# Three edits to the expert routing of a fused attention, gated FFN and expert kernel: second tile gathered early, second expert fixed early, router matrix turned once

## The reference

```
x = attention(q, k, v)            # 4 batches x 8 heads, 576 tokens, block-causal mask (blocks of 64)
x = (sigmoid(x @ w_gate) * (x @ w_val)) @ w_out        # 512 -> 1536 -> 512
logits = x @ router                                     # 2304 x 8
expert_idx = argmax(logits)
gate_w = softmax(logits)[expert_idx]
for e in range(8):
    mask = expert_idx == e
    h = maximum(x[mask] @ w1[e], 0)                     # 512 -> 1024
    out[mask] = gate_w[mask] * (h @ w2[e])              # 1024 -> 512
```

## Time and profile before

| what | us |
|---|---|
| median of 3 runs | 953.57 |
| the profiled execution | 957.25 |
| its span, first to last instruction | 955.5 |
| PE busy | 899.2 (94%) |
| DVE / ACT / POOL busy | 515.7 / 298.2 / 273.7 |
| mean granted PE clock | 0.976 of 2.4 GHz |

### The profile page before, as it was taken

The page is one execution under the profiler, slowest core; times in us unless marked ns, Lnnn a source line. Parts: engine busy times, 40 slices in busy tenths (PEclk is TensorE's granted clock), DMA queues, the critical chain, the costliest instruction groups (busy, mean ns, idle before and its releaser), DMA issues.

```text
span 955.5 us, 15628 instructions
## 1 busy us (share of the span) xinstructions
PE 899.2 (94%) x5198; PEld 742.0 (78%) x5199; DVE 515.7 (54%) x1027; ACT 298.2 (31%) x672; POOL 273.7 (29%) x254
## 2 busy tenths in 40 slices
PE   7989898999999999999999999799878999989995
PEld 3545454589999999999999999698667888878884
DVE  5777676741248549638747746933543435362241
ACT  4555455532231121121122112123132424351140
POOL 4133335321112213212212212123043435452242
PEclk9999999999999999999999999899798999989998
DMA  4544455422230020010002000022144336382130
GB/s 133 160 158 159 157 171 165 146 95 78 77 122 1 1 67 1 1 34 34 1 1 67 1 1 34 28 94 85 51 168 149 130 132 210 113 276 70 44 132 28
DMA packets 48089, 85.29 MB, mean 89 GB/s; under 512 B 9247, under 2 KB 21535, under 8 KB 47904
## 3 DMA queue, kind: packets, MB, share of 16 engines
q1 hardware_dynamic: 42272, 69.32, 22.1%
q0 software_dynamic: 3360, 10.50, 3.4%
q10 hardware_dynamic: 2400, 4.72, 1.4%
HBM read 70.28 MB, written 14.76 MB: 89 GB/s over the span
## 4 chain that ended last, share of the span: by engine, by line
PE 73%; DMA 8%; DVE 7%; issue 5%; POOL 2%; ACT 2%; SPq 1%; POOLq 0%; DVEq 0%; ACTq 0%
PE bank L1383 21%; PE bank L1385 20%; PE bank L1384 20%; DMA rinv_scratch<-rinv 3%; PE bank L1355 3%; PE bank L1316 3%; PE bank L1328 3%; DMA rwide<-rinv_scratch 2%; PE bank L1518 2%; POOL w1l L436 2%; DVE yT L1021 2%; DMA stage<-in_we 2%; DVE bank L1021 1%; DVE nmax L971 1%; PE bank L1486 1%
## 5 line engine op out<-in xcount | busy, mean ns | idle before, releaser
L689 POOL TENSOR_TENSOR hl<-hraw,hh 128x384 fp32r<-128x384 f32 x72 | 93.7, 1302 | 366.4 <-ACT hh L826 366.4
L1383 PE MATMUL bank<-xh,w1h 128*128 128x384 f32 x576 | 195.6, 340 | 2.0 <-DVE hraw L1143 2.0
L1385 PE MATMUL bank<-xh,w1l 128*128 128x384 f32 x576 | 194.5, 338 | 0.0
L1384 PE MATMUL bank<-xl,w1h 128*128 128x384 f32 x576 | 194.3, 337 | 0.0
L1143 DVE TENSOR_TENSOR hraw<-hraw,bank 128x384 f32<-128x384 f32 x72 | 39.8, 553 | 178.8 <-ACT hraw L871 178.3
L1383 PEld LDWEIGHTS bank<-xh,w1h 128*128 128x128 f32 x576 | 109.4, 190 | 4.8 <-DVE hraw L1143 2.5
L1384 PEld LDWEIGHTS bank<-xl,w1h 128*128 128x128 f32 x576 | 109.4, 190 | 2.2
L1385 PEld LDWEIGHTS bank<-xh,w1l 128*128 128x128 f32 x576 | 109.2, 190 | 0.0
L797 ACT ACTIVATE prob<-bank,nmax 128x576 f32<-128x576 f32 (+2 forms) x144 | 75.9, 528 | 89.4 <-DVE nmax L971 86.4
L871 ACT ACTIVATE hraw<-bank 128x384 f32<-128x384 f32 x72 | 35.4, 491 | 216.3 <-PE bank L1385 216.3
L1021 DVE CUSTOM_DVE_ANT_0 yT<-yrow,wrb 128x512 f32<-128x512 f32 x60 | 89.3, 1488 | 0.0
(11 more groups left out here) (184 smaller groups left out, 1420.5 us busy)
## 6 DMA issues: line engine op xcount, KB each, us to landing
stage<-in_we SPq DMA_DIRECT2D x56, 512.0 KB, 4.4
w1raw<-in_w SPq DMA_DIRECT2D x8, 768.0 KB, 4.6
kt<-in_kT SPq DMA_DIRECT2D x16, 288.0 KB, 3.4
qt<-in_qT SPq DMA_DIRECT2D x16, 288.0 KB, 3.8
rwide<-rinv_scratch SPq DMA_DIRECT2D x32, 144.0 KB, 3.0
xt_scratch<-xo SPq DMA_DIRECT2D x16, 288.0 KB, 2.2
xraw<-xt_scratch SPq DMA_DIRECT2D x6, 768.0 KB, 4.6
y_scratch<-yrow ACTq DMA_DIRECT2D x6, 768.0 KB, 5.0
```

What stands on the lines that cost most here:

```text
L689: pool.tensor_tensor(hl[:, f % 2, :], hraw[:, f % 2, :], hh[:, f % 2, :].bitcast(F32), ALU.subtract).then_inc(h_low, 1)
L1383: pe.matmul(out_, wh, ah, start=first, stop=False, skip_group_check=True)
L1384: pe.matmul(out_, wh, al, start=False, stop=False, skip_group_check=True)
L1385: return pe.matmul(out_, wl, ah, start=False, stop=last, skip_group_check=True)
```

## The change

1. **Router matrix turned once.** wrb becomes [8, 512]. In group 0 SP loads four pieces of 128x1024 (one after each of the w_out blocks 7 to 10) into the still unused yrow, and POOL copies each into wrb with the two axes exchanged, in steps 8 to 11 (`wrb_turn`). Each piece waits for the copy of the one before, as they share one place.
2. **One dense order of routing** for all groups: logits 3, 3, 6, 6, 6 in steps 0 to 4, `routes` in 5, `ranks` in 6, `slots` in 7, `table` in 8, `add_table` in 9. So `first_expert` (17 small operations instead of 13) moves from step 10 of group 4 to step 7.
3. **Second tile early.** After group 4's tokens are in the table, the first expert's second column is looked up too (`first_rows(1)`), and POOL gathers tile 1 in step 10 of group 5. Its rows get their own split buffers ygh1 and ygl1. Should the expert have fewer than 256 rows by then, the column stays as it is and later rows go to the next one (`filled`).
4. **Second expert fixed early** as the first of the ascending order; its weights are requested right behind those of the first one. It gets at least one tile.
5. **The start of the expert part is written out** for tiles 0 and 1, in halves (`up_half`), with matmuls of tile 1 in the places where PE waited for tile 0's hidden rows; ACT does both relus there.
6. **In `over_loads`** the eighth block of the next load moves behind the load's second tile (`second_step`), or into an Else branch where there is none (`rest`).

```diff
-    NT = TT + E - 1
+    NT = TT + E
-        wrb = sb(s2, "wrb", [P, D, E])
+        wrb = sb(s2, "wrb", [P, E, D])
-        def route_steps(G):
-            if G == G_LAST:
-                return [0, 4, 8, 16, 24], 4, 5, 6, 7
-            return [3 * f for f in range(9)], 8, 9, 10, 11
+        LOGIT_STEP = [0, 3, 6, 12, 18, 24]
+        HOT_STEP, RANK_STEP, SLOT_STEP, TAB_STEP = 5, 6, 7, 8
+        ROWS0_STEP, GATHER1_STEP = 9, 10
...
+                if WRB_STEP <= k < WRB_STEP + 4:
+                    j = k - WRB_STEP
+                    if j:
+                        sp.wait_ge(wrb_made, j)
+                    sp.dma_start(yrow[:].rearrange("p m d -> p (m d)")[:, 0:WD * E],
...
+            def wrb_turn(j):
+                pool.wait_ge(wrb_loaded, 16 * (j + 1))
+                pool.tensor_copy(wrb[:, :, j * WD:(j + 1) * WD],
+                                 yrow[:].rearrange("p m d -> p (m d)")[:, 0:WD * E].rearrange("p (d e) -> p e d", e=E)
+                                 ).then_inc(wrb_made, 1)
...
                     hlow(G, f)
+                    if G == 0 and WRB_STEP < f <= WRB_STEP + 4:
+                        wrb_turn(f - WRB_STEP - 1)
                     if G == G_LAST:
                         if f == 1:
+                            early_gather(0)
                         weights_low(pool, 0, 0, LOW_POOL_STEP.get(f, []), ew_low_p)
+                        if f == GATHER1_STEP:
+                            early_gather(1)
             pool.wait_ge(second_known, 1)
-            pool.wait_ge(ygT_done, 1)
+            pool.wait_ge(ygT_done, 2)
...
-            gather(1)
+            gather(2)
+            weights_low(pool, 1, 1, LOW_POOL[:2], ew_low_p)
             pool.wait_ge(tables, 1)
             columns(0)
-            pool.wait_ge(tables, 2)
-            gather_ahead(0)
+            gather_ahead(1)
+            scatter(1)
+            pool.wait_ge(out_stored, 16)
+            columns(1)
...
-                    dve.tensor_tensor_reduce(junk, yrow[:, m, :], wrb[:, :, e], 1.0, 0.0, ALU.mult, ALU.add,
+                    dve.tensor_tensor_reduce(junk, yrow[:, m, :], wrb[:, e, :], 1.0, 0.0, ALU.mult, ALU.add,
...
+            up_half(0, 0, [0, 1])
             for m in range(GM):
                 turn_y(GM * G_LAST + m, m)
+            turn_rows(1)
             for m in range(GM):
                 router(m)
-            expert_up(0, 0, 0)
+            up_half(0, 0, [2, 3]).then_inc(el1_half, 1)
+            up_half(0, 1, [0, 1])
+            ranks(G_LAST)
+            up_half(0, 1, [2, 3]).then_inc(el1_done, 1)
+            pe.wait_ge(yg_high, 2)
+            pe.wait_ge(yg_low, 2)
+            pe.wait_ge(hrow_a, 1)
+            up_half(1, 0, [0, 1])
             turn_hidden(0)
+            up_half(1, 0, [2, 3])
             table(G_LAST)
+            up_half(1, 1, range(C)).then_inc(el1_done, 1)
             expert_down(0, 0, 1)
-            turn_rows(1)
+            turn_rows(2)
+            turn_hidden(1)
             pe.wait_ge(loads_known, 1)
-            over_loads(pe, first_step, step)
+            over_loads(pe, first_step, step, step)
```

More of the change, by code:

```diff
@@ L436, in weights_low, with over_loads, from_second @@
                 eng.tensor_tensor(lo, stage_at(k), h.bitcast(F32), ALU.subtract).then_inc(made, 1)
[L438 removed]
+        def over_loads(eng, first_step, second_step, step, rest=None):
+            def from_second(l, par, t, t1):
+                with eng.If(t1 > t):
+                    second_step(l, par, t)
+                    with eng.If(t1 > t + 1):
+                        with eng.Fori(t + 1, t1) as u:
+                            step(l, par, u)
+                if rest is not None:
+                    with eng.Else():
+                        rest(l, par)
             def load(l, par):
@@ L444, in load @@
                 if isinstance(l, int) and l == 0:
[L445 to L448, removed]
+                    from_second(0, 0, 2, t1)
                     return
@@ L874, in group @@
                         act.copy(woh[:, f, :], woraw[:, f % 2, :]).then_inc(wo_high, 1)
-                    if not first and f == route_steps(G)[2]:
+                    if not first and f == RANK_STEP:
                         lsigmoid(G - 1)
@@ L889, in _, with hidden_high @@
             yout(NG - 1)
[L890 to L901, removed]
+            def hidden_high(t):
                 act.wait_ge(hT_done, t + 1)
-                if not zero:
+                if not (isinstance(t, int) and t == 0):
                     act.wait_ge(el2_done, t)
@@ L906, in hidden @@
                          ).then_inc(hT_high, 1)
+            def hidden(t):
+                act.wait_ge(el1_done, t + 1)
+                act.wait_ge(hT_done, t)
+                act.activation(hrow[:, 0:512], bank[0][:, 0, :], ACT.Relu).then_inc(hrow_a, 1)
+                rows_high(t + 1)
+                hidden_high(t)
             def first_step(l, par, t):
[L909 to L912, removed]
                 act.wait_ge(el1_done, t)
@@ L1502, in expert_up, with up_half @@
                     for half in range(2):
-                        if zero and c == 1 and half == 1:
-                            ranks(G_LAST)
-                        wh, wl = ew1_at(par, c, half)
-                        last = three(bank[0][:, half, :], ygh[:, c, :], ygl[:, c, :], wh, wl, c == 0, c == C - 1)
+                        last = up_of(t, par, c, half, c == 0, c == C - 1)
                 last.then_inc(el1_done, 1)
+            def up_half(t, half, cs):
+                for c in cs:
+                    last = up_of(t, 0, c, half, c == 0, c == C - 1)
+                return last
             def turn_hidden(t):
@@ L1537, in first_step @@
                 turn_rows(t + 1)
-                if not (isinstance(l, int) and l == 0):
-                    expert_down(l - 1, 1 - par, t)
+                expert_down(l - 1, 1 - par, t)
                 turn_hidden(t)
```

245 lines of the change are left out of this document (152 added, 93 removed).

## The result

| | this kernel | the kernel before |
|---|---|---|
| median of 20 runs, us | 946.41 (943.43 to 953.37) | 955.86 (951.02 to 964.48) |
| profiled execution, us | 945.51 | 957.25 |
| its span, us | 943.7 | 955.5 |
| mean granted PE clock, of 2.4 GHz | 0.983 | 0.976 |

The ratio of the two is 0.9903, with a 95% interval from 0.9884 to 0.9922: the kernel is faster by 1%, where 1.9% was forecast (935.6 us, range 927 to 946). The time lies 0.4 us above the range.

The account below looks back on a forecast made before the run. PE, busy 94%, was taken to lose time only by waiting or running below full clock. Terms -10.3 - 0.5 - 15.6 + 0.8 + 7.6 = -18.0 from the median 953.57 gave 935.6 us, range 927 to 946.

Parts of the forecast that it names:

- The start of the expert part: From the last group's end to tile 3's turn_hidden: 53.0 us where it was 68.57, term -15.6 us.
- DVE has the four tables (7 us) ahead of tile 2's low part: PE waits 0.8: Start of the expert part, after tile 0's down: DVE's table work delays tile 2's rows, PE waits only 0.8 us.
- Group 0: Router-matrix pieces, POOL copies, w_out blocks and hl form one chain of rounds: stall 5.2 plus low clock, +7.6 us.
- d: Duration of one POOL copy of a router-matrix piece in group 0, taken as 1.9 us; the stall is 3d - 0.5.
- Dense routing: Last group's waits and low clock go, -10.3 us; the earlier first_expert in group 4 gives -0.5 us.
- the group loses nothing either way: Last group: even with slow logits DVE ends at 33.4 us, before hraw is needed at 35.5; groups 1 to 4 don't gain.
- Loads with one tile: Expert part near 835 us: the eighth block waits for the scatter and comes 0.5 to 1.5 us later, +0.8 us.
- Early second tile, second expert, tile count: Last group and expert part: tile 1 gathered early, second expert's blocks cast before needed, 20 tiles with none added.
- The second: Start of the expert part: POOL comes last for tiles 2 to 5, 7 to 8 of 15.6 us lost, 943 us; chance 0.2.
- The first: Group 0: the chain is free, copy of 1.04 us and no fall of the clock, 930.6 us; chance 0.2.
- the third: Group 0: slower than before through a slow copy, which would have to take 7.9 us; chance 0.04.
- The fourth: Last group: tile 1's gather is held up in step 10 and doesn't come early, some 6 us lost, 941 us; chance 0.05.

Follow-up runs that it names:

- both edits: Changed kernel with router-matrix pieces after w_out blocks 4, 6, 8, 10 and POOL's blocks 1 and 3 of the second expert behind the scatter: 930.46 us, 0.9708.
- the other pair: Changed kernel with router-matrix pieces spaced out (936.67 us) against changed kernel with POOL's two second-expert subtractions behind the scatter (938.29 us).
- both doses: Changed kernel with two POOL weight-block subtractions ahead of the tables (946.41 us), or only one, the other behind the scatter (943.68 us).
- one block: Changed kernel with block 1 of the second expert left ahead of the tables on POOL, block 3 moved behind the scatter: 943.68 us, 0.9857.
- the two single edits: Changed kernel with only POOL's two second-expert subtractions moved behind the scatter (938.29 us), or only the router-matrix pieces spaced out (936.67 us).
- the blocks moved: Changed kernel with POOL's subtractions of blocks 1 and 3 of the second expert behind tile 3's gather and tile 0's scatter: 938.29 us, 0.9798.
- the pieces spread: Changed kernel with the four router-matrix pieces requested after w_out blocks 4, 6, 8 and 10 in place of 7 to 10: 936.67 us, 0.9783.

## Why the prediction was wrong

**The start of the expert part (the step that failed).** The step "DVE has the four tables (7 us) ahead of tile 2's low part: PE waits 0.8" took DVE's time from instructions that ran undisturbed. The change puts two subtractions of 2.4 us on POOL just where DVE builds the load table, and the prediction asked only what stands behind them in POOL's queue (tile 3's gather, 1.0 late) and not what DVE is doing meanwhile. DVE was held for 5.2 us; with its low clock this costs 7.7 us (57.1 against 49.4 in the kernel with both edits, which has the same clock ahead of it; 55.4 against 47.8 for the other pair). That is more than the whole miss of 5.3 in this stretch: without it the stretch would have been 50.6 from the group's end, and the prediction's 53.0 was 2.4 too high, mostly in the router and `up`, of which less ran at the low clock than it counted (it had turn_hidden(0) 15.1 us after the group's end, it came after 13.1). Without the 7.7 the median would have been 938.7, inside the range; so this one wait made the miss, and luck of the other sign hid a part of it. The trace of before had the sign: logits of 1.2 us that took up to 2.03 when POOL worked. The prediction used it for the logits and not here.

The Trainium skill (SBUF — State Buffer, "Who interferes with whom") says that DVE and GpSimd share one pair of SBUF ports as an exclusive lock, which is held for a whole instruction. This agrees with sel, a comparison with two SBUF inputs, which ends 0.1 us after POOL's subtraction in both doses; the row of two back-to-back subtractions adds that DVE didn't get in between them. That sel's row begins 0.63 us ahead of the subtraction's isn't explained by it.

**Group 0: right in mechanism, too small.** The chain, the place and the engine were as forecast. It was 9.9 and not 7.6: 7.7 of waits for hl and 2.1 of clock (79.53 busy against 77.39). d was 2.2 and not 1.9, and a round 8.7 to 9.1 and not 7.9: beside d a round had 6.5 to 6.9 where 6.0 were counted, mostly because the w_out block behind a piece landed 4.3 us after the copy's end (257.6 to 261.9) and not 3.6. With the chain gone the copies took as long (2.17) and cost nothing, so the links made the price.

**Dense routing: the sum right, its reason wrong.** Group 5 gave 10.7 for 10.3 and group 4 its 0.5. But "the group loses nothing either way" doesn't hold, as the unturned matrix shows: 3.7 in group 5 and 7.9 in groups 1 to 4. The prediction asked when hraw is due, 35.5 us after the group's first sigmoid, and not when the one-hot rows are. In group 5 of the unturned kernel DVE has the last logit and the hraw behind it done after 35.2 us (forecast 33.4), in time for PE. But the seven small operations up to the one-hot rows end after 37.3, and PE is free for `ranks` after 35.4: the wait of 1.9. In the dense order `ranks` of groups 1 to 4 stands in step 6 and no longer in 9, behind as many logits, and the order alone in the kernel before brought the same five waits. Which part of it makes them, the denser logits or the earlier `ranks`, wasn't tried apart.

**Loads with one tile.** Forecast +0.8, measured 0.1 to 0.3: the relu of the place that waits at 835 us comes 112.56 us after turn_hidden(3), and before it was 112.48; PE goes on there after 114.1 us, and before after 113.8. The stretch as a whole is 0.9 shorter, at clock 0.98 against 0.97.

**Early second tile, second expert, tile count.** As forecast: the gather is issued in group 5 and makes nobody wait, no weight block is waited for after the group, and there are 20 tiles.

**The rivals.** The second (943 us, the start gives half back) came nearest in number, and it blamed POOL. But its mechanism, gathers that come late because POOL is the last in order, didn't occur: PE waits for no gather among tiles 2 to 6. The first (a free chain) and the third (a copy of 7.9 us) are refuted by the copy's 2.2. The fourth didn't occur. Against the first stood "the clock fell after each wait above 2 us"; this isn't so even in the trace of before, as the last section shows, though it did fall in group 0.

**The numbers.** From 935.6 to 946.4 are 10.8 us: 6.2 from the terms above, 2.3 because the three runs of before had a median of 953.57 and the twenty have 955.86, and the other 2.3 because the profiled executions stood 1.4 above and 0.9 below their medians. Two readings of the prediction are off without weight for the sum: the row of 75.67 us that it calls group 4's is group 3's (group 4 is the 76.16 that it uses later), and its "about 6" for the window at 827 us comes out with three tiles of 12.3 and not with 3.5.

Open stays why the router part ahead of turn_hidden(0) takes 11.9 us in some kernels (the changed one, both edits, one block, the matrix not turned) and 10.3 at full clock in others (the two single edits, the blocks moved and the pieces spread). It wasn't tried apart; by this much two single runs can differ there.

## What to carry to other kernels

When work is moved onto GpSimd, look at what VectorE does in the same microseconds, and not only at the queue behind the moved work: a short instruction on the path, with both inputs in SBUF, took as long here as GpSimd's block. Where two queues and two engines each wait for the other's last step, give the loop two steps of time per round; the same four copies then cost nothing here. And a denser order is worth what the slowest instruction in it allows, so it is to be timed together with the edit that makes this instruction short.

## What the runs showed of the hardware

- A DVE tensor_tensor of 72 elements took 0.23, 3.13 and 5.44 us beside none, one and two POOL subtractions of 128x1024, and two in a row held it to the end of the second. In the kernel with the blocks moved a DVE operation whose inputs are a PSUM bank and one SBUF tile took its usual 0.69 while POOL's subtractions ran (695.55 to 700.41):

```profile
698.36 0.69 DVE L1204 TENSOR_TENSOR ygl<-bank,ygh 128x512 fp32r<-128x512 f32 x1 [0.41 <-ACT ygh L903]
```

- POOL's copy of 128x1024 that reads at 32 bytes took 2.17 us (2.12 to 2.38 in the changed kernel); by its contiguous cast 0.98 would be expected, an estimate, as a contiguous copy wasn't run, so the step seems to more than double it. The Trainium skill (GPSIMD Engine Reference, Performance pitfalls for Q7 kernels) has half as much again for such reads, which would be an estimate of 1.5; the measurement decides.
- The length of PE's wait alone didn't tell the clock behind it. After 1.4 us, for ygl in the two kernels with the blocks moved, PE went on at full clock (0.23 us a matmul of 512 columns); after 4.3, 6.7 and 7.0 us it went on at 0.43, the lower level, for 9 to 12 of them. Between these the same wait had either outcome: the low level after 1.7 and 1.9 us for the one-hot rows of the unturned kernel, the full one after 3.2 us near 829 us with the blocks moved, the low one after 3.2 us near 848 us before. The wait for hTl near the end, in the kernel before and in the one with both edits:

```profile
941.25 0.49 PE L1383 MATMUL bank<-ew2h,hTh 128*128 128x512 f32 x1 [3.02 <-DVE hTl L1266]
941.58 0.40 PE L1384 MATMUL bank<-ew2l,hTh 128*128 128x512 f32 x1
```

```profile
916.92 0.79 PE L1469 MATMUL bank<-ew2h,hTh 128*128 128x512 f32 x1 [3.04 <-DVE hTl L1337]
917.51 0.63 PE L1470 MATMUL bank<-ew2l,hTh 128*128 128x512 f32 x1
```
